# Two fp32 feed-forward layers behind windowed attention: tiles of 256 tokens, double FFN chunks and two sets of accumulators

## The reference

```
scores = q @ k.T / sqrt(64)               # 4 sequences, 8 heads, 576 positions, head width 64
scores = where(0 <= row - col < 64, scores, -1e9)
attn   = exp(scores - max) / (sum + 1e-9)
x = (attn @ v) as [2304 tokens, 512]
x = relu(x @ moe_w_in) ** 2 @ moe_w_out    # 512 -> 2048 -> 512
h = x @ moe2_w_in
out = (h * cos(h)) @ moe2_w_out            # 512 -> 2048 -> 512
```

## Time and profile before

| | |
|---|---|
| three runs | 919.89, 920.98, 922.46 us, median 920.98 |
| profiled execution: span from first to last instruction | 921.4 us, inside the range of the three; no other time was taken for it |
| PE, PEld busy | 895.2 us, 850.5 us |
| DVE, ACT, POOL busy | 529.7, 359.8, 152.8 us |
| DMA | 54.68 MB, mean 59 GB/s |

### The profile page before, as it was taken

How to read it: one execution, slowest core, us unless ns; L and a number is a source line. 1 busy time by engine, 2 the same in 40 slices (tenths; PEclk the granted TensorE clock), 3 DMA queues, 4 the chain that set the end, 5 groups by cost and what they waited for, 6 DMA issues and landing times.

```text
span 921.4 us, 14725 instructions
## 1 busy us (share of the span) xinstructions
PE 895.2 (97%) x5040; PEld 850.5 (92%) x5040; DVE 529.7 (57%) x986; ACT 359.8 (39%) x903; POOL 152.8 (17%) x119
## 2 busy tenths in 40 slices
PE   6899999999999999999989999999999999999998
PEld 6899999999999999999989889889989988889997
DVE  6676744434434443443588866665665765766665
ACT  5444344434434443443212333433433333343433
POOL 3565500001000000000387310000000100100000
PEclk9999999999999999999999999999999999999999
DMA  6555402211211221100444310010000010000000
GB/s 194 156 153 142 141 37 66 77 63 36 78 57 40 79 57 63 56 29 0 149 115 129 112 35 1 34 34 0 34 34 0 34 34 0 34 0 0 35 1 35
DMA packets 57119, 54.68 MB, mean 59 GB/s; under 512 B 22592, under 2 KB 40512, under 8 KB 57088
## 3 DMA queue, kind: packets, MB, share of 16 engines
q1 hardware_dynamic: 56560, 54.15, 19.4%
q10 hardware_dynamic: 528, 0.13, 0.1%
HBM read 44.83 MB, written 9.44 MB: 59 GB/s over the span
## 4 chain that ended last, share of the span: by engine, by line
PE 78%; DVE 8%; DMA 5%; ACT 3%; issue 3%; POOL 2%; SPq 1%; DVEq 0%; ACTq 0%
PE h L371 26%; PE y L427 20%; PE y L401 15%; PE turned L371 5%; PE scores L371 4%; DMA w_raw<-w_out 3%; PE turned L361 2%; PE scores L333 2%; DVE work L731 2%; POOL w_in_lo L855 2%; ACT arena L496 1%; PE turned L346 1%; DVE work L690 1%; DVE g_lo L695 1%; DVE w_in_hi L683 1%
## 5 line engine op out<-in xcount | busy, mean ns | idle before, releaser
L371 PE MATMUL h<-x_hi,w_in_hi 128*128 (+1 forms) x576 | 199.3, 346 | 1.7 <-DVE x_lo L665 1.7
L371 PE MATMUL h<-x_hi,w_in_lo 128*128 (+1 forms) x576 | 193.9, 337 | 0.0
L371 PE MATMUL h<-x_lo,w_in_hi 128*128 (+1 forms) x576 | 193.7, 336 | 0.0
L695 DVE TENSOR_TENSOR g_lo<-work,g_hi 128x384 fp32r<-128x384 f32 x192 | 115.1, 600 | 126.4 <-ACT g_hi L533 126.4
L533 ACT CAST g_hi<-work 128x384 fp32r<-128x384 f32 x192 | 97.3, 507 | 137.5 <-PE y L401 69.3
L401 PE MATMUL y<-g_hi,w_out_hi 128*128 128x384 f32 x384 | 129.0, 336 | 2.4 <-DVE g_lo L695 2.4
L401 PE MATMUL y<-g_lo,w_out_hi 128*128 128x384 f32 x384 | 129.0, 336 | 0.0
L401 PE MATMUL y<-g_hi,w_out_lo 128*128 128x384 f32 x384 | 129.0, 336 | 0.0
L427 PE MATMUL y<-w_out_hi,g_hi 128*128 128x512 f32 x288 | 112.8, 392 | 7.3 <-DVE g_lo L695 5.0
L427 PE MATMUL y<-w_out_hi,g_lo 128*128 128x512 f32 x288 | 113.9, 395 | 0.0
L427 PE MATMUL y<-w_out_lo,g_hi 128*128 128x512 f32 x288 | 113.7, 395 | 0.0
(11 more groups left out here) (96 smaller groups left out, 1295.5 us busy)
## 6 DMA issues: line engine op xcount, KB each, us to landing
arena<-k_cols SPq DMA_DIRECT2D x33, 256.0 KB, 3.4
arena<-v_rows SPq DMA_DIRECT2D x33, 256.0 KB, 3.5
w_raw<-w_in SPq DMA_DIRECT2D x32, 256.0 KB, 2.9
w_raw<-w_out SPq DMA_DIRECT2D x32, 256.0 KB, 2.6
x_tiles<-work SPq DMA_DIRECT2D x6, 768.0 KB, 3.3
arena<-x_tiles SPq DMA_DIRECT2D x6, 768.0 KB, 4.3
arena<-q_blocks SPq DMA_DIRECT2D x68, 64.0 KB, 2.4
out<-work SPq DMA_DIRECT2D x5, 768.0 KB, 3.5
```

The costliest lines, as they stand in the source:

```text
L371: mm = pe.matmul(bank[:, 0:TILE], w[:, k, cols], x_at(x, par, k), start=(n == 0), stop=(n == 3 * KC - 1))
L695: nc.vector.tensor_tensor(g_lo[:, f % 2, :], act[:, f % 2, :], g_hi[:, f % 2, :].bitcast(fp32), ALU.subtract).then_inc(glo_set, 1)
```

## The change

It rewrites the schedule.

- Tiles are of 256 tokens, 9 of them, four blocks each. Two hidden chunks share a PSUM bank, 2 x 256 columns: a step s is a double chunk, 8 steps a tile. `up` makes 24 matmuls of 256 columns, `down1` 24 of 256, `down2` 12 of 512. The operations of ACT and DVE between them work on 512 columns instead of 384.
- Layer 1's four output parts share two banks; the four y banks are two sets, taken in turn by tile.
- In layer 1 ACT makes g_hi from relu by Square (`g_high1`), and DVE squares in place beside it.
- A tile's result is stored as two words, high by ACT (`y_high`), low by DVE (`y_low`), and layer 2 loads both straight into x_hi and x_lo.
- POOL keeps masks, the first four norms and three weight pieces. The other norms are on DVE. Weight pieces are of 128 x 1024; ACT casts the high word (`w_high`), DVE subtracts the low one (`w_low`).
- q comes with its zeros from the host, q, k and v by two blocks at a time (duo), k and v repeated where windows overlap; two slots.
- PE's list per step: up1, in an odd step pv, the down1 of the step before, in an even step turn, in an odd step qk of the next block. In layer 2 down2 stands two steps behind up2, and the scalar and vector lists begin a step with g_high2 and g_low of the step before.
- All loops are unrolled. ACT's table for the sine is loaded by an instruction of its own at the end of layer 1.

```diff
-    TILE = 384
+    STEPS = w_in1.shape[0]
+    TILE = 256
     TILES = TOKENS // TILE
     QT = TILE // BLK
     TB = TILE // P
-    LAG = 2
...
-        y_bank = [ps(f"y{d}") for d in range(KC)]
-        s_bank = ps("scores")
-        t_bank = ps("turned")
+        s_bank, t_bank = ps("scores"), ps("turned")
+        y_bank = [ps(f"y{n}") for n in range(4)]
...
+        pieces = [("in", 0)] + [(kind, s - (kind == "out")) for s in range(1, STEPS) for kind in ("in", "out")]
+        pieces += [("out", STEPS - 1)]
+        PIECES = len(pieces)
+        EARLY = 3
         number = {what: n for n, what in enumerate(pieces)}
-        EARLY = 6
 
...
+
+            return [n for n in (number.get(("in", step + 2)), number.get(("out", step + 1))) if n is not None]
 
+                    if n is not None]
 
...
+                sp.dma_start(x2_dram[j], stage[:, :, :]).then_inc(stored, 16)
+
...
+                slot = (TILES + j) % 2
+                sp.wait_ge(up_done, STEPS * (TILES + j - 1))
+                sp.wait_ge(stored, 16 * (j + 1))
+                sp.dma_start(x_hi[:, slot].bitcast(fp32), x2_dram[j, :, 0].rearrange("p (k c) -> p k c", k=KC))\
                   .then_inc(x2_loaded, 16)
-
+                  .then_inc(x2_loaded, 16)
+
...
+            sp.dma_start(q_at[0], q_duos[0]).then_inc(qk_loaded[0], 16)
+            load_qk(1)
+            load_v(0)
+            load_piece(0)
+            load_v(1)
+            load_piece(1)
+            load_piece(2)
+            load_qk(2)
+            load_v(2)
+            load_qk(3)
+            load_piece(3)
+            load_v(3)
+            load_piece(4)
+            for s in range(STEPS):
+                for n in pieces_of(s + 1):
                     load_piece(n)
+                    load_qk(4)
+                    load_v(4)
+            load_qk(5)
+            load_v(5)
+            for j in range(1, TILES):
...
+            def up(s, slot, bank):
+                for f in range(2):
                     cols = slice(f * P, (f + 1) * P)
-                    for w, x in ((w_in_hi, x_hi), (w_in_hi, x_lo), (w_in_lo, x_hi)):
-                        mm = pe.matmul(bank[:, 0:TILE], w[:, k, cols], x_at(x, par, k),
-                                       start=(n == 0), stop=(n == 3 * KC - 1))
-                        n += 1
+                    n = 0
+                    for k in range(KC):
+                        for w, x in ((w_in_hi, x_hi), (w_in_hi, x_lo), (w_in_lo, x_hi)):
+                            mm = pe.matmul(bank[:, f * TILE:(f + 1) * TILE], w[:, s, k, cols], x[:, slot, k, :],
+                                           start=(n == 0), stop=(n == 3 * KC - 1))
+                            n += 1
...
+            def down1(j, s):
+                g = j * STEPS + s
+                pe.wait_ge(glo_set, g + 1)
+                if j == 0:
+                    weights_split(number["out", s])
+                if s == 0 and j >= 2:
+                    pe.wait_ge(ylo_set, 2 * (j - 1))
                 for d in range(KC):
-                    cols = slice(d * P, (d + 1) * P)
+                    bank = y_bank[2 * (j % 2) + d // 2]
+                    for f in range(2):
+                        for n, (w, x) in enumerate(((w_out_hi, g_hi), (w_out_hi, g_lo), (w_out_lo, g_hi))):
+                            mm = pe.matmul(bank[:, d % 2 * TILE:(d % 2 + 1) * TILE], w[:, s, f, d * P:(d + 1) * P],
+                                           x[:, g % 2, f * TILE:(f + 1) * TILE],
+                                           start=(s == 0 and f == 0 and n == 0 and d % 2 == 0),
+                                           stop=(s == STEPS - 1 and f == 1 and n == 2), skip_group_check=True)
                 mm.then_inc(down_done, 1)
...
+            def down2(j, s):
+                g = j * STEPS + s
+                t = TILES + j
+                pe.wait_ge(glo_set, L2 + g + 1)
+                if j == 0:
+                    weights_split(PIECES + number["out", s])
+                if s == 0:
+                    if j < 2:
+                        pe.wait_ge(ylo_set, 2 * (t - 1))
+                    else:
+                        for b in range(TB):
+                            pe.wait_ge(y2_copied[b], j - 1)
                 for b in range(TB):
+                    bank = y_bank[2 * (t % 2) + b]
+                    for f in range(2):
+                        cols = slice(f * TILE + b * P, f * TILE + (b + 1) * P)
+                        for n, (x, w) in enumerate(((g_hi, w_out_hi), (g_hi, w_out_lo), (g_lo, w_out_hi))):
+                            mm = pe.matmul(bank[:, :], x[:, g % 2, cols], w[:, s, f, :],
+                                           start=(s == 0 and f == 0 and n == 0),
+                                           stop=(s == STEPS - 1 and f == 1 and n == 2))
+                    if s == STEPS - 1:
+                        mm.then_inc(down_done, 1)
+                if s < STEPS - 1:
                     mm.then_inc(down_done, 1)
...
+            qk(QT)
+            for j in range(TILES):
+                for s in range(STEPS):
+                    t = QT * (j + 1) + s // 2
+                    up1(j, s)
+                    if s % 2 == 1 and t < NBLK:
+                        pv(t)
+                    if s > 0:
+                        down1(j, s - 1)
+                    elif j > 0:
+                        down1(j - 1, STEPS - 1)
+                    if s % 2 == 0 and t < NBLK:
+                        turn(t)
+                    if s % 2 == 1 and t + 1 < NBLK:
+                        qk(t + 1)
+            for j in range(TILES):
+                for s in range(STEPS):
+                    g = j * STEPS + s
+                    up2(j, s)
+                    if g == 0:
+                        down1(TILES - 1, STEPS - 1)
+                    if g >= 2:
+                        down2((g - 2) // STEPS, (g - 2) % STEPS)
+            down2(TILES - 1, STEPS - 2)
+            down2(TILES - 1, STEPS - 1)
...
+            def w_high(n):
+                _, hi, _, raw = piece(n)
+                kind, s = pieces[n % PIECES]
+                act_e.wait_ge(w_loaded[n % WSLOTS], 16 * (n // WSLOTS + 1))
+                if n >= PIECES:
+                    act_e.wait_ge(up_done if kind == "in" else down_done, L2 - STEPS + s + 1)
+                nc.scalar.copy(hi, raw).then_inc(whi_set, 1)
+
+            def relu(g):
+                act_e.wait_ge(up_done, g + 1)
+                if g >= 2:
+                    act_e.wait_ge(glo_set, g - 1)
+                nc.scalar.activation(act[:, g % 2, :], h_bank[g % 2][:, :], ACT.Relu).then_inc(relu_set, 1)
+
+            def g_high1(g):
+                act_e.wait_ge(relu_set, g + 1)
+                if g >= 2:
+                    act_e.wait_ge(down_done, g - 1)
+                nc.scalar.activation(g_hi[:, g % 2, :], act[:, g % 2, :], ACT.Square).then_inc(ghi_set, 1)
...
+            def y_high(j):
+                act_e.wait_ge(down_done, STEPS * (j + 1))
+                if j > 0:
                     act_e.wait_ge(stored, 16 * j)
                 for b in range(2):
-                    nc.scalar.copy(y_stage[:, b * D:(b + 1) * D], y_bank[b][:, :]).then_inc(y_copied, 1)
+                    nc.scalar.copy(stage[:, 0, b * 2 * TILE:(b + 1) * 2 * TILE].bitcast(f32r),
+                                   y_bank[2 * (j % 2) + b][:, :]).then_inc(yhi_set, 1)
...
+            for j in range(TILES):
+                for s in range(STEPS):
+                    g = j * STEPS + s
+                    t = QT * (j + 1) + s // 2
+                    if j == TILES - 1:
+                        for n in pieces2_of(s):
+                            w_high(n)
+                    if s % 2 == 0 and t < NBLK:
+                        exps(t)
+                    if s % 2 == 1 and t < NBLK:
+                        copy_turned(t)
+                    if j == 0:
+                        for n in pieces_of(s):
+                            w_high(n)
+                    relu(g)
+                    g_high1(g)
+                    if s % 2 == 1 and t < NBLK:
+                        x_high(t)
+                    if s == 0 and j > 0:
+                        y_high(j - 1)
+            nc.scalar.activation(warm[:, :], warm[:, :], ACT.Sin).then_inc(warmed, 1)
...
+                    g = j * STEPS + s
+                    if g > 0:
+                        g_high2(g - 1)
+                    if g < 2:
+                        for n in pieces2_of(STEPS + g):
+                            w_high(n)
+                    count_turns(g)
+                    if g == 0:
+                        y_high(TILES - 1)
+                    if s == 2 and j > 0:
+                        y2_copy(j - 1)
+                    cosines(g)
+            g_high2(L2 - 1)
+            y2_copy(TILES - 1)
...
+            def norm(t):
+                dve.wait_ge(inverted, t + 1)
+                inv = inv_sum[:, t % QT, :].rearrange("p (a o) -> p a o", o=1)
```

(134 more changed lines are left out.)

792 lines of the change are left out of this document (252 added, 540 removed).

## The result

The changed kernel took 965.21 us (median of 4 runs, 964.45 to 966.82), the kernel before 921.72 beside it (4 runs, 919.89 to 922.70): ratio 1.0475, 95% interval 1.0452 to 1.0497. The direction is the one predicted, the size is not: 936 was forecast, in a range up to 952.

The account below looks back on a forecast made before the run. TensorE, 97% busy, was taken as the bound. Stalls removed -18, matmuls and prologue 0, turn waits +18, first tile +12.7, clock +1.7, last down2 +0.15: +15 on 921.4, 936 us; own range 926 to 946, 8-in-10 range 912 to 952.

Parts of the forecast that it names:

- Turn comes too early: PE's turn waits for VectorE's norm, 0.65 us in each of 28 blocks of tiles 1 to 7: +18 us.
- the first tile: Weight casts in the chain before turn make its waits longer, 5.4, 2.8, 2.8 and 1.7 us: +12.7 us.
- Stalls removed: Waits of down2, down1 and turn, the low clock and hidden parts of waits go: -18 us together.
- Rival 2: Turn doesn't wait, as operations or hops at 512 columns are cheaper than scaled: 918 or 912 us; chance 0.10.
- Prologue and blocks put inside: First up at 27, -3 us; attention blocks moved behind it, +3.6; net 0, between -3 and +4.
- I take 0.1157, since both nearest rows lie at 0.45 ns a column: change 0: Up and down1: 256-column matmuls cost 0.1157 us each, in proportion to 384 columns; change 0, ends -35 and +22 us.
- own sign of being wrong, over 0.119: The prediction called itself wrong if a 256-column matmul took under 0.112 or over 0.119 us.
- the high end (0.120): Upper price of a 256-column matmul in up and down1, with a fixed 0.0135 us in each: +22 us.
- rival 3: A fixed cost per matmul makes 256 columns take 0.120 us: +22 less 7, 951 us; chance 0.08.
- Loads ... Nothing; a late load would show as a wait of scores: DMA loads of attention inputs, weights and x2 add no time; a late one would show at PE's scores.
- Clock: TensorE's clock may fall after the first tile's stop of 5.4 us: +1.7 us.
- Layer 2's round: Scalar and vector round of 4.7 us stays under PE's 5.56 per step; becoming the bound, 961 us, had chance 0.04.

Follow-up runs that it names:

- Experiment 2: Changed kernel with VectorE's invert and norm moved from behind square to right behind the maximum: 931.66 us, ratio 1.0104 to the kernel before.
- experiment 7: Kernel before with GpSimd's x2_low issued as four operations of 384 columns instead of one of 1536: 916.64 us, ratio 0.9947.
- experiment 6: Kernel before with x2_low alone moved from GpSimd to VectorE, right behind the cast: 916.94 us, ratio 0.9935.
- Experiment 1: Changed kernel with layer 2's first three weight pieces issued ahead of the last store of x2: 955.75 us, ratio 1.0366 to the kernel before.
- experiment 8: Kernel before, GpSimd out of the splits: from the seventh piece high words on ScalarE, low words on VectorE; x2_low on VectorE: 911.07 us, ratio 0.9880.
- experiment 5: Changed kernel with pieces issued early, norm first, and each 512-column down2 matmul split into two of 256: 932.02 us, ratio 1.0110 to the kernel before.

## Why the prediction was partly right and where it failed

- **Turn comes too early: right.** 30.7 us for all 32 were predicted, 30.6 measured; 0.65 a block against 0.63. The end of norm was off by 0.17, which down1's cover made up: 48 x 0.0043 = 0.2 longer. The two errors cancel, and so do those of the first tile (5.4, 2.8, 2.8, 1.7 against 6.29, 2.55, 2.55, 1.57): that the sums agree to 0.1 us is in part luck. Experiment 2 shows the mechanism: moving norm alone takes the waits away.
- **Stalls removed: right, 0.9 too large.** -15.4 in waits and -1.7 for the old clock stretch that the prediction knew are -17.1 against -18. 0.8 of the waits that it summed is the turn's for GpSimd at 23.4, ahead of the first up, and so counted once more in its prologue. And x2_low made at most part of down1's wait: of its 2.4 us 1.9 stay with x2_low in four parts (experiment 7) and 1.0 with none of it on GpSimd (experiment 6). A second stretch of before (30.0 to 33.4, another 1.7) it had missed. Rival 2, no wait of turn, is refuted.
- **Prologue and blocks put inside: 3.9 off.** 0 was predicted and -4.8 + 0.9 = -3.9 came, below its range of -3 to +4: the first up was at 25.1, not 27, and the blocks inside cost 0.9 more, not 3.6.
- **"I take 0.1157, since both nearest rows lie at 0.45 ns a column: change 0": failed, +20.9.** The 0.230 of the earlier trace rows made the law look proportional: 0.1735/384 and 0.230/512 are both 0.45 ns. Alone, 512 columns take 0.2267, on the line 13.3 ns + N / 2.4 GHz through 384. Six starts in a stretch where other engines were busy stood for a price that rested on a difference of 3 ns; before's last matmuls, 35 distances from 909.79 to 917.76 or 0.2277 each, would have shown it. The prediction's own sign of being wrong, over 0.119, is met. The right value was worked out as the high end (0.120) and as rival 3, and given a chance of 0.08. Why 512 columns take 0.229 to 0.231 in the mean inside the kernels, against 0.2267 alone, isn't settled.
- **"Loads ... Nothing; a late load would show as a wait of scores": failed, +7.3, and 2.1 of clock.** I counted bytes and time between loads, and not what stands ahead of a piece in SyncE's list, where a store that waits for y_low was the item to see. Nor did it show at scores: an in-order ScalarE passed it on to g_low and so to down1. Experiment 1 shows it.
- **Clock: 1.7 predicted, 5.2 lost**: 1.55 each at the turns' waits of 6.3 and 2.6 in the first tile and 2.1 behind down1's. Net of the second old stretch 3.5. Waits of 0.6 us never brought it down.
- **Layer 2's round**: did not bind, as predicted; down2 waits 0.1 us in all.

By these terms: 936 + 20.9 (matmuls) + 7.3 (late piece) + (3.5 - 1.7) (clock) - 3.9 (prologue and blocks) + 0.9 (stalls removed) - 0.2 (turns, and a last down2 that hardly waited) = 962.8; the span is 962.7.

The change as a whole buys 19 us of stalls (15.4 of waits, 3.4 of clock) and 4 us of prologue with 21 us of matmuls, and loses the rest by the order of two lists. With these in order it is level. All waits of down1 and down2 went at 384 columns too (experiment 8, 10.9 us faster than the kernel before), without the extra matmuls and with one set of accumulators, so neither the smaller tile nor the second set was needed for them. Storing x2 in two words and q's zeros from the host were not tested by themselves.

## What to carry to other kernels

Count matmuls, not only columns: at 256 and 384 columns each had a fixed part here (13.3 ns), so 1728 more of them cost 21 to 23 us; take such a price from a long undisturbed row of starts. For every in-order list, DMA issues included, write down what stands between the producer and its consumer: a norm behind a square, a weight load behind a store and a cast that waits for a DMA ahead of a relu cost 43 us here, and reordering alone gave them back. An operation that may wait belongs at the end of a round, where the least that PE soon needs stands behind it.

## What was not expected of the hardware

- 128 and 192 columns cost the same, 111 and 111.7 ns between starts, though their columns alone would be 53 and 80 ns. With weights of 64 columns instead of 128, 256 columns take 113.3 ns instead of 120.0, and 384 take 173.3 either way.
- 448 columns take 206.7 ns, 7 more than the line through its neighbours.
- Loads' own records are 188 to 193 ns long while pairs start every 111 to 120. Loads are 98% busy in experiment 5 and 90% in the changed kernel, at the same 120 ns a pair of 256 columns, so their busy share didn't give the price.
- In or just behind waits of 1.7 to 7.2 us the granted clock stood at 1.2 GHz for 3.4, 6.8 or once 10.2 us (experiment 2). Which of them followed no pattern that these runs show, nor did it always fall: of two waits of 2.39 us in the changed kernel's first tile, at 52.15 and 68.48, only the second brought it down.
